# Expert choice of two batches moved from GpSimd to VectorE, and the bonus rows from VectorE to ScalarE

## What is computed

```
for t in range(S):                          # per batch b and head h
    cur = u[None] * kt (outer) vt           # the bonus of the token itself
    y[:, :, t] = rt . (state + cur)
    state = wt * state + kt (outer) vt

logits = x @ w_gate;  noise_scale = log1p(exp(x @ w_noise))
top2 = the two largest of logits + noise_scale * noise
out[token] += weight_k * (relu(x @ w1[e]) @ w2[e])      for both chosen e

h = x @ w_in;  out = (h - tanh(h)) @ w_out
```

## Time and profile before

| | |
|---|---|
| median of 3 runs | 1154.87 us (1149.25 to 1158.71) |
| the profiled execution's own time | 1149.97 us |
| its span | 1148.1 us |
| PE busy, share of span | 1084.0 us, 94% |
| DVE | 705.2 us, 61% |
| ACT | 548.8 us, 48% |
| POOL | 193.7 us, 17% |

### The profile page before, as it was taken

The page is one execution under the profiler, slowest core; times in us unless marked ns, Lnnn a source line. Parts: engine busy times, 40 slices in busy tenths (PEclk is TensorE's granted clock), DMA queues, the critical chain, the costliest instruction groups (busy, mean ns, idle before and its releaser), DMA issues.

```text
span 1148.1 us, 24038 instructions
## 1 busy us (share of the span) xinstructions
PE 1084.0 (94%) x8735; PEld 1038.2 (90%) x8735; DVE 705.2 (61%) x913; ACT 548.8 (48%) x757; POOL 193.7 (17%) x317
## 2 busy tenths in 40 slices
PE   4987968799999999999999999999999999999999
PEld 4776857788999999999999999899999999999998
DVE  8978676468977777777777777543434334343432
ACT  4444331545557767777766766423232323323232
POOL 2108575145800000000000000401010110101000
PEclk8899697899999999999999999999999999999999
DMA  7645352677878888888888888402010110101000
GB/s 129 143 117 126 110 131 94 222 246 253 272 240 301 291 285 286 290 296 281 275 282 291 293 295 289 136 18 62 1 62 0 62 35 26 62 0 62 0 21 21
DMA packets 120719, 183.86 MB, mean 160 GB/s; under 512 B 12112, under 2 KB 84048, under 8 KB 120656
## 3 DMA queue, kind: packets, MB, share of 16 engines
q1 hardware_dynamic: 106048, 152.44, 42.8%
q0 software_dynamic: 6144, 18.88, 5.0%
q10 hardware_dynamic: 8464, 11.70, 2.9%
HBM read 155.67 MB, written 27.33 MB: 159 GB/s over the span
## 4 chain that ended last, share of the span: by engine, by line
PE 80%; DVE 7%; POOL 5%; issue 3%; ACT 2%; DMA 2%; another core or an unknown queue 1%; SPq 0%; POOLq 0%; ACTq 0%; DVEq 0%
PE ps L861 6%; PE ps L862 6%; PE ps L863 6%; PE ps L879 6%; PE ps L880 6%; PE ps L881 6%; PE ps L789 6%; PE ps L785 6%; PE ps L786 6%; PE ps L736 4%; PE ps L745 4%; PE ps L737 4%; DVE w_lo L1566 2%; PE ps L761 2%; PE ps L762 2%
## 5 line engine op out<-in xcount | busy, mean ns | idle before, releaser
L1566 DVE TENSOR_TENSOR w_lo<-w_raw,w_hi 128x1536 fp32r<-128x1536 f32 x140 | 243.3, 1755 | 58.1 <-ACT w_hi L935 57.2
L935 ACT ACTIVATE w_hi<-w_raw 128x1536 fp32r<-128x1536 f32 x140 | 204.5, 1483 | 43.6 <-PE ps L789 43.6
L1990 POOL DMA_INDIRECT yy<-yg,slot_g x48 | 48.1, 1002 | 687.9 <-DVE w_lo L1566 408.9
L1566 DVE TENSOR_TENSOR gg<-ps,th 128x768 f32<-128x768 f32 x64 | 61.3, 957 | 167.3 <-ACT th L1174 167.3
L785 PE MATMUL ps<-w_hi,h_hi 128*128 128x384 f32 x440 | 152.5, 347 | 0.3
L789 PE MATMUL ps<-w_hi,h_lo 128*128 128x384 f32 x440 | 149.4, 340 | 0.8 <-issue 0.7
L786 PE MATMUL ps<-w_lo,h_hi 128*128 128x384 f32 x440 | 147.9, 336 | 2.0 <-issue 2.0
L861 PE MATMUL ps<-x2T_hi,win_hi 128*128 128x384 f32 x384 | 128.3, 334 | 1.1 <-DVE x2T_lo L1566 1.1
L863 PE MATMUL ps<-x2T_hi,win_lo 128*128 128x384 f32 x384 | 128.3, 334 | 0.0
L862 PE MATMUL ps<-x2T_lo,win_hi 128*128 128x384 f32 x384 | 128.3, 334 | 0.0
L879 PE MATMUL ps<-wout_hi,g_hi 128*128 128x384 f32 x378 | 128.2, 339 | 0.0
(11 more groups left out here) (292 smaller groups left out, 2067.3 us busy)
## 6 DMA issues: line engine op xcount, KB each, us to landing
w_raw<-in_moe_w SPq DMA_DIRECT2D x140, 768.0 KB
xt_in<-xg SPq DMA_DIRECT2D x20, 384.0 KB, 5.9
yg<-y_out ACTq DMA_DIRECT2D x20, 384.0 KB
klin<-in_k_cols SPq DMA_DIRECT2D x32, 144.0 KB, 3.8
v_nat<-in_v_pairs SPq DMA_DIRECT2D x16, 288.0 KB, 3.1
wz<-in_w_cols SPq DMA_DIRECT2D x30, 144.0 KB, 3.6
rlin<-in_r_cols SPq DMA_DIRECT2D x28, 144.0 KB, 3.7
out<-o_out SPq DMA_DIRECT2D x7, 576.0 KB
```

Source lines behind the costliest of these rows:

```text
L935: nc.scalar.activation(dst, src, ACT.Copy).then_inc(s, 1)
L1566: vec.tensor_tensor(dst, a, b, ALU.subtract).then_inc(s, 1)
```

## The change

It has three parts. (1) `bonus` leaves DVE. ACT copies the 12 numbers per token of `betas` out of PSUM (`beta`) and forms the bonus rows by 12 copies of 128x48, each scaled by one column; for this `betas` write to another PSUM bank, with a semaphore `betas_full`. (2) On PE `add_bonus` stands behind `inter`. (3) The choices of batches 0 and 1, and their slots, run on DVE by the functions that batches 2 and 3 use, one pair or more apart; a batch takes `softplus_1` to `softplus_3` (4 instructions), `choose_1` and `choose_2` (8 each) and `slots` (5), each behind the one before by a semaphore. POOL keeps `finish` and `scatter`; all tables are moved to suit.

```diff
-        BETA = D * Q
+        BETA = QT * P
@@ def betas(p):
-                follow(pe, S_ready, p)
+                pe.wait_ge(back_copied[1], p + 1)
+                follow(pe, beta_s, p)
-                        pe.matmul(ps[rows, KV, BETA + 2 * q:BETA + 2 * q + D], ...
+                        mm = pe.matmul(ps[rows, T1, BETA + 2 * q:BETA + 2 * q + D], ...
+                mm.then_inc(betas_full, 1)
@@ PE's pair
+                inter(p)
                 add_bonus(p)
-                inter(p)
@@ PE's table
-                     (8, 2): [turns(1, 0, 0)], (8, 3): [lambda: ranks(0, xTr_ready, 2 * KD + 1)], (9, 0): [turns(1, 0, 1)], ...
+                     (7, 2): [lambda: ranks(0, lg_taken, 1)],
+                     (8, 2): [turns(1, 0, 0)], (9, 0): [turns(1, 0, 1)], (9, 1): [turns(1, 0, 2)],
-                     (13, 0): [lambda: ranks(1, lg_taken, 2)],
+                     (12, 0): [lambda: ranks(1, lg_taken, 2)],
@@ ACT
+            def bonus(p):
+                act.wait_ge(v_in_s[p % 2], 16 * (p // 2 + 1))
+                act.wait_ge(betas_full, p + 1)
+                follow(act, Y_full, p)
+                cp(beta[:], ps[0:C, T1, BETA:BETA + 2 * Q], beta_s)
+                act.wait_ge(beta_s, p + 1)
+                for q in range(Q):
+                    for h in range(2):
+                        nc.scalar.activation(bv[:, q, h, :], v_nat[p % 2][:, q, h, :], ACT.Copy,
+                                             scale=beta[:, 2 * q + h:2 * q + h + 1]).then_inc(bv_done, 1)
@@ ACT's pair
                 step(p, 0)
+                bonus(p)
                 chunk_products(p + 2)
@@ DVE's table
-            steps = {(6, 0): [lambda: take(0)], (9, 0): [lambda: placed(0)], (10, 0): [lambda: weights(0)], (10, 1): [lambda: take(1)],
-                     (13, 4): [lambda: placed(1)], (13, 1): [early_1], (13, 3): [early_2], (14, 3): [lambda: weights(1)],
+            steps = {(6, 0): [lambda: take(0), lambda: softplus_1(0)], (6, 4): [lambda: softplus_2(0)], (6, 1): [lambda: softplus_3(0)],
+                     (6, 3): [lambda: choose_1(0)], (7, 4): [lambda: choose_2(0)], (8, 0): [lambda: placed(0), lambda: slots(0)], (8, 1): [lambda: weights(0)],
+                     (10, 1): [lambda: take(1), lambda: softplus_1(1)], (10, 3): [lambda: softplus_2(1)], (11, 4): [lambda: softplus_3(1)],
+                     (11, 1): [lambda: choose_1(1)], (11, 3): [lambda: choose_2(1)], (12, 1): [lambda: placed(1), lambda: slots(1)], (12, 3): [early_1],
+                     (13, 1): [early_2], (13, 3): [lambda: weights(1)],
@@ POOL
-            noisy(0)
-            choices(0)
             finish(1)
-            chosen(0)
-            slots(0)
+            scatter(0, 0, 4, 17)
             range_part(2)
-            scatter(0, 0, 4, 18)
```

More of the change, by code:

```diff
@@ L557, in betas @@
                         rows = slice(half * HB, (half + 1) * HB)
-                        pe.matmul(ps[rows, KV, BETA + 2 * q:BETA + 2 * q + D], kr[:, q * C + half * HB:q * C + (half + 1) * HB],
+                        mm = pe.matmul(ps[rows, T1, BETA + 2 * q:BETA + 2 * q + D], kr[:, q * C + half * HB:q * C + (half + 1) * HB],
                                   usel[:, p % HP, :], start=True, stop=True, skip_group_check=True)
+                mm.then_inc(betas_full, 1)
             def back(p):
@@ L566, in back @@
                     follow(pe, back_copied[half], p)
+                    if half == 1:
+                        follow(pe, beta_s, p)
                     for j in range(QT):
@@ L575, in outer @@
                 s = p % 2
+                follow(pe, S_ready, p)
                 pe.wait_ge(v_in_s[s], 16 * (p // 2 + 1))
@@ L602, in add_bonus @@
             def add_bonus(p):
-                pe.wait_ge(bv_done, p + 1)
+                pe.wait_ge(bv_done, 2 * Q * (p + 1))
                 for h in range(2):
-                    pe.matmul(ps[:, Y0 + h, 0:Q * D], ident[:], bv[:, :, h, :], start=False, stop=True, skip_group_check=True)
+                    mm = pe.matmul(ps[:, Y0 + h, 0:Q * D], ident[:], bv[:, :, h, :], start=False, stop=True, skip_group_check=True)
+                mm.then_inc(Y_full, 1)
             def inter(p):
@@ L616, in inter @@
                             rows = slice(half * HB, (half + 1) * HB)
-                            mm = pe.matmul(ps[rows, Y0 + h, q * D:(q + 1) * D],
+                            pe.matmul(ps[rows, Y0 + h, q * D:(q + 1) * D],
                                            rPW[s][keys, q * C + half * HB:q * C + (half + 1) * HB], Zall[keys, :, q - 1],
                                            start=False, stop=True, skip_group_check=True)
-                mm.then_inc(Y_full, 1)
             def turn_rows(c, hf, kk, bank, reader, value):
@@ L632, in rows_in_turn @@
                 n = 2 * KD * c + KD * hf + kk
-                read = {(0, 0, 0): (setup, 0), (1, 0, 0): (lg_taken, 1), (1, 0, 1): (rank_read, 2), (2, 0, 0): (rank_read, 4),
-                        (3, 0, 0): (lg_taken, 3)}
+                read = {(0, 0, 0): (setup, 0), (1, 0, 0): (rank_read, 2), (2, 0, 0): (rank_read, 4), (3, 0, 0): (lg_taken, 3)}
                 turn_rows(c, hf, kk, row_bank(c, n), *read.get((c, hf, kk), (xTr_ready, n - (c == B - 1))))
@@ L1610, in _ @@
                 decayed_r(p + 1)
-                bonus(p)
                 if p % HP == 2:
@@ L1905, in chosen @@
-            def chosen(ci):
-                nG = groups(ci)[1]
-                a, b, d = t1[:, 0:nG], t2[:, 0:nG], t3[:, 0:nG]
-                follow(po, weighed, 2 * ci)
-                for m, oh in ((m1, oh1), (m2, oh2)):
-                    seq(po.tensor_tensor(b, oh[:, 0:nG], a, ALU.mult))
-                    total_of(m[:, 0:nG], b, d)
-                told(po.tensor_tensor(m2[:, 0:nG], m2[:, 0:nG], m1[:, 0:nG], ALU.subtract), z_ready, 4 * ci + 4)
-            def slots(ci):
-                gs, nG = groups(ci)
-                a, b, d = ranked[:, 0:nG], t2[:, 0:nG], t3[:, 0:nG]
-                po.wait_ge(rank_read, 2 * ci + 2)
-                for kk, oh in enumerate((oh1, oh2)):
-                    seq(po.tensor_tensor(b, oh[:, 0:nG], a, ALU.mult))
-                    total_of(slot_f[:, gs, kk], b, d)
-                told(po.tensor_copy(slot_now[:, gs, :], slot_f[:, gs, :]), slots_ready, ci + 1)
@@ L1937, in _ @@
             range_part(1)
-            noisy(0)
-            choices(0)
             finish(1)
-            chosen(0)
-            slots(0)
+            scatter(0, 0, 4, 17)
             range_part(2)
-            scatter(0, 0, 4, 18)
-            scatter(0, 4, 8, 21)
-            noisy(1)
-            scatter(0, 8, 12, 23)
-            choices(1)
+            scatter(0, 4, 8, 20)
+            scatter(0, 8, 12, 22)
             finish(2)
-            chosen(1)
-            slots(1)
             range_part(3)
-            scatter(1, 0, 4, 28)
-            scatter(1, 4, 8, 30)
-            scatter(1, 8, 12, 31)
+            scatter(1, 0, 4, 26)
+            scatter(1, 4, 8, 28)
+            scatter(1, 8, 12, 30)
             finish(3)
```

67 lines of the change are left out of this document (10 added, 57 removed).

## The result

| | before | changed |
|---|---|---|
| median of 17 runs each | 1151.87 us | 1145.44 us |
| profiled execution, its span | 1149.97, 1148.1 us | 1143.71, 1142.1 us |
| ratio | | 0.9945 (95% interval 0.9926 to 0.9964) |
| DVE, ACT, POOL busy | 705.2, 548.8, 193.7 us | 704.3, 594.0, 144.2 us |

The change is worth 6.4 us where 17.9 were forecast. 1145 lies inside the range, but the forecast of its size was wrong. On the profiled execution the span is 6.0 us shorter.

The account below looks back on a forecast made before the run. No engine was full in the attention; DVE bounded pairs and waited 13.1 us for counts behind POOL's choice. Segments A to F summed to 202.7 against 220.57 us, 17.9 less, giving 1137 us; range 1125 to 1150.

Parts of the forecast that it names:

- C: Attention from mask(0) of pair 9 to mask(0) of pair 11: 33.4 us before, forecast 21.4, bounds 18.2 and 26.4.
- D: Attention from mask(0) of pair 11 to mask(0) of pair 13: 19.1 us before, forecast 27.0, with routing work added.
- E: Attention from mask(0) of pair 13 to mask(0) of pair 14: 24.0 us before with a wait of 8.31, forecast 11.5.
- F': Stretch from mask(0) of pair 14 to the last mask, used for comparing profiles; it had no forecast of its own.
- F: From mask(0) of pair 14 to the first expert matmul: 35.15 us before, forecast 27.3 at full clock, bounds 22.4 and 35.15.
- A: From the start to take(0), 82.17 us before: forecast 1.0 us more, bounds -3.3 and +1.5.
- B: From take(0) to mask(0) of pair 9: 26.7 us before, forecast 32.3, three bonuses off and 33 routing instructions on.
- rival 3: DVE merely swaps bonus work for routing work and the 13.1 us of waits for counts stay: 1156 us, chance 0.06.
- Rival 4: ACT becomes the loop through the bonus copies: at 0.5 us a copy a pair takes 10.9, 1166 us, chance 0.06.
- Rival 1: More comes back: ACT stall gone, early pairs gain bonuses, no slow clock in C; typical gain 25, 1130 us, chance 0.18.
- The rule that it leaned on: Skill text that instruction refills are mostly hidden: the 4.91 us ACT stall would be chance and F 22.4.
- Rival 2: Waits handed on: C and F stay at upper bounds through turns, logits and loads, not POOL; 1150 us, chance 0.20.

## Why the prediction was wrong

**The step that failed** is one sentence on POOL: "Small waits are priced at nothing on POOL: ... and scatters hide under the pairs that follow." They hide from POOL's side, but in the profiled changed kernel they cost 12.8 us behind take(0), 5.0 of it in C, 1.0 in D, 0.3 in E and 6.5 in F', partly through the lower clock behind a stall. Of the 11.5 us by which the gain fell short, 9.4 lie in the attention (212.06 for 202.7) and 2.5 behind it (the profiled executions gained 6.0, the medians 6.4). Where they cost nothing, the sum was good to 3.5 us: on the chip without stalls the changed kernel's segments are 81.62, 34.10, 22.96, 26.73, 11.45 and 22.39, first expert matmul 199.25, against 202.7 forecast. The same costs stood in the time of before, and I booked them as gain to come: by the profiles, C's 33.4 had 3.7 of them and F's 35.15 had 10.3 up to the last mask, of which the clock may hold a part. E's 24.0 had 4.4, and only these the change takes away, with POOL's choice. I compared a kernel with scatters in its way to a sum without. Where they don't stall PE, the sum comes true and the gain still doesn't: 1124.32 and 1121.03 us, 3.3 and not 17.9.

**A**, 81.88 for 83.2: inside its bounds, and as argued the first pairs kept none of their saved bonuses. **B**, 34.10 for 32.3: 1.75 us are the wait for the count, which comes as rival 3's arithmetic had it, "at the same time", within 2 us; it stood in every changed kernel (1.6 to 2.4). **C**, 27.78 for 21.4: beyond even the upper bound of 26.4, the mis-sized term. That bound was priced as a low clock through the logits. The clock over C was 0.87, and 0.99 with late scatters: it fell during PE's pauses, to 0.50 from 139.2 to 141.6 us. **D**, 27.77 for 27.0, and **E**, 11.66 for 11.5: the price of 0.24 us a routing instruction and of the moved table parts holds. **F**, 28.87 for 27.3, looks like a hit and is two errors that cancel. The clock did rise, from 0.76 to 0.93, as I reckoned; the unnamed ACT stall of 4.91 us that I kept lies over a group of scatters (200.25 to 205.00) and is in none of the three profiles of the kernel before with late scatters. In its place the changed kernel lost 6.5 in F'. Without them F is 22.39, the lower bound of my range for it.

**After the attention** I had nothing: all was to move with its end. 2.5 us were given back there, and the clock has 2.3 of them. PE does the same matmuls in the same order in both. 1.4 us go in the first 3 us of the expert tiles, where the granted clock is 0.50 (212.0 to 215.3) and 1.00 at that place before, and 0.9 at 731.5 to 734.0, 0.50 for 1.00 again.

**The bonus on ACT** went as forecast: ACT's timeline of pair 3 and DVE's from mask to mask show it.

```profile
47.20 0.18 ACT L941 ACTIVATE beta<-ps 128x12 f32<-128x12 f32 x1 [1.11 <-PE ps L560]
47.41 2.82 ACT L1006 ACTIVATE bv<-v_nat,beta 128x48 f32<-128x48 f32 x12
50.43 0.63 ACT L994 ACTIVATE Wx<-Gz 128x240 f32<-128x240 f32 x1 [0.20 <-DVE Zall L1572]
```

```profile
44.02 0.94 DVE L1563 TENSOR_TENSOR Am<-ps,before 128x768 f32<-128x768 f32 x1
...
52.76 0.95 DVE L1563 TENSOR_TENSOR Am<-ps,before 128x768 f32<-128x768 f32 x1
```

Twelve copies take 2.82 us, 0.235 each for 0.23 forecast; Wx is released by Zall; the pair is 8.74 us for 8.75. Rival 4 is out. **Rival 1** had F right (22.4) where no scatter interferes: the ACT stall isn't there, though instructions are fetched there too (the DMA rows from 132 to 141 us have two packets of them). The rule that it leaned on agrees with that; no run tests more of it. **Rival 2** came nearest in time (1150), had C right, and its sign, unnamed stalls after pair 14, was there; but F didn't stay at its upper bound (28.87 for 35.15), and it named turns, logits and loads as the cause, where it was POOL. **Rival 3** has the balance right once the scatters are out of the way: the change ends within 2 us of where it began. Its mechanism is not what happened, since the waits don't stay: the change swaps 16 bonuses and most of two waits of 4.8 and 4.0 us for routing work. I gave it 0.06, since I had taken the 13.1 us of waits for what POOL's arithmetic costs.

## What to carry over

Before you book an idle stretch as the gain of a change, ask what else makes it long: here half of a wait of 8.3 us, and up to 10 of the 24 us from mask(0) of pair 14 to the last mask, came from scatters, which the change leaves in place. A stretch that the profile puts down to "issue" or "remote" on two engines at once deserves a look at what POOL issues at that time. If transfers by list must stand in the loop, the places where DVE bounds it and nobody waits for PE are the first to try. And time a pair of kernels on one chip, with the old kernel as a candidate of its own, before you trust half a per cent.

## What the runs showed of the chip

While POOL issued scatters by lists of 128 rows, PE passed its small products in bursts of 1 to 5 every 0.72 us without waiting for any engine, for up to 4 us a group of four, and its granted clock was 0.50 for a while behind that. 64 bytes a row did it as much as 1536, plain copies of 1536 didn't. The first two profiles and those of three more sets show this, each set on another chip. Those of the remaining two sets, on two further chips, don't: one with the changed kernel itself, the other only with its scatters in other places. Not every group does it: that at 109 us of the changed kernel did not, that at 121 us made one pause of 0.28 us, and there the scatters themselves were long, up to 2.50 and 1.86 us for 0.96 (the profile without stalls has such long ones too, up to 2.50). The 48 gathers from 716 us on, beside matmuls of larger tiles, made none. No packet of instructions starts in the two stalls looked at. What PE and POOL share there, no row shows, and it stays open.
